# Attention with a sliding window and two MLPs on one core: the second set of weight combinations moves from POOL to VectorE and ACT, four products move between the last pairs' work, and VectorE takes sums first at changes of super-block

## The reference, cut to what matters

```python
# attention: 4 batches, 8 heads, 576 positions, head size 64
scores = scale * np.matmul(q, k.transpose(0, 1, 3, 2))
mask = (rel >= 0) & (rel < 128)
scores = np.where(mask, scores + bias[None], -1000000000.0)
attn = np.exp(scores - max); attn = attn / (sum + 1e-09)
x = np.matmul(attn, v)               # as 2304 tokens x 512
# first MLP: w_in 512 x 2048, w_out 2048 x 512
h = np.maximum(x @ w_in, 0.0); x = h * h @ w_out
# second MLP
h = x @ w_in; out = (h * np.cos(h)) @ w_out
```

## Time and profile before

| | before |
|---|---|
| median of 3 runs | 881.16 us (880.2 to 881.41) |
| the profiled execution's own time | 880.24 us |
| its span | 878.4 us |
| PE busy | 850.0 us (97%) |
| DVE busy | 645.3 us (73%) |
| ACT busy | 522.7 us (60%) |
| POOL busy | 96.1 us (11%) |
| granted clock of PE | 1.0 throughout |

### The profile page before, as it was taken

How to read it: one execution, slowest core, us unless ns; L and a number is a source line. 1 busy time by engine, 2 the same in 40 slices (tenths; PEclk the granted TensorE clock), 3 DMA queues, 4 the chain that set the end, 5 groups by cost and what they waited for, 6 DMA issues and landing times.

```text
span 878.4 us, 16151 instructions
## 1 busy us (share of the span) xinstructions
PE 850.0 (97%) x5840; PEld 766.0 (87%) x5840; DVE 645.3 (73%) x1437; ACT 522.7 (60%) x1141; POOL 96.1 (11%) x193
## 2 busy tenths in 40 slices
PE   6998789999999999999999999999999999999997
PEld 4887688999989999989999988898889889898986
DVE  6899577876767857777676687776777777767664
ACT  7888533433343433243342687887787877877774
POOL 7799900000000000000000000000000000000000
PEclk9999999999999999999999999999999999999999
DMA  6877506456588777777877556555575555565522
GB/s 211 254 236 264 184 12 229 155 209 239 181 293 297 235 283 287 276 243 284 297 265 256 190 194 202 183 163 187 187 264 181 168 190 192 204 224 183 192 72 72
DMA packets 72047, 185.34 MB, mean 211 GB/s; under 512 B 7200, under 2 KB 19488, under 8 KB 69920
## 3 DMA queue, kind: packets, MB, share of 16 engines
q1 hardware_dynamic: 71104, 183.23, 60.8%
q10 hardware_dynamic: 864, 1.08, 0.3%
HBM read 141.82 MB, written 42.47 MB: 210 GB/s over the span
## 4 chain that ended last, share of the span: by engine, by line
PE 87%; DVE 7%; issue 2%; POOL 2%; ACT 1%; DMA 0%; ACTq 0%; DVEq 0%; POOLq 0%
PE psum L699 38%; PE psum L733 22%; PE psum L738 14%; PE psum L740 7%; PE psum L642 2%; PE psum L554 2%; POOL probs L492 1%; PE psum L600 1%; DVE probs L1057 1%; DVE guarded L1066 1%; DVE g_lo L1231 1%; DVE hidden_sum L1177 1%; DVE pt L1077 1%; ACT probs L805 0%; DVE x L1101 0%
## 5 line engine op out<-in xcount | busy, mean ns | idle before, releaser
L699 PE MATMUL psum<-xt_hi,comb 128*128 128x384 f32 x1344 | 396.3, 337 | 6.2 <-DVE hidden_sum L1177 6.1
L699 PEld LDWEIGHTS psum<-xt_hi,comb 128*128 128x128 f32 x1344 | 247.4, 188 | 22.9 <-issue 8.2
L733 PE MATMUL psum<-wout,g_hi 128*128 128x512 f32 x576 | 180.5, 394 | 1.6 <-issue 1.3
L902 ACT ACTIVATE g_hi<-work 128x384 fp32r<-128x384 f32 x192 | 97.2, 518 | 95.2 <-DVE work L1226 53.9
L738 PE MATMUL psum<-g_hi,wout 128*128 128x512 f32 x384 | 149.7, 393 | 0.0
L1231 DVE TENSOR_TENSOR g_lo<-work,g_hi 128x384 fp32r<-128x384 f32 x192 | 102.1, 552 | 45.5 <-ACT g_hi L902 44.4
L699 PE MATMUL psum<-x_lo,comb 128*128 128x384 f32 x384 | 129.0, 336 | 0.0
L733 PEld LDWEIGHTS psum<-wout,g_hi 128*128 128x128 f32 x576 | 105.8, 188 | 14.6 <-issue 2.9
L733 PE MATMUL psum<-wout,g_lo 128*128 128x512 f32 x288 | 113.9, 395 | 0.0
L740 PE MATMUL psum<-g_hi,wout 128*128 128x256 f32 x384 | 107.9, 281 | 0.0
L699 PE MATMUL psum<-xt_lo,comb 128*128 128x384 f32 x288 | 96.9, 336 | 0.0
(11 more groups left out here) (101 smaller groups left out, 1292.7 us busy)
## 6 DMA issues: line engine op xcount, KB each, us to landing
comb<-comb SPq DMA_DIRECT2D x80, 768.0 KB, 4.9
wout<-wout SPq DMA_DIRECT2D x48, 512.0 KB, 4.9
comb<-comb SPq DMA_DIRECT2D x8, 1792.0 KB, 6.7
comb<-kept SPq DMA_DIRECT2D x8, 1792.0 KB, 7.4
wout_raw<-w_out SPq DMA_DIRECT2D x48, 256.0 KB, 4.4
comb<-comb SPq DMA_DIRECT2D x40, 256.0 KB, 3.1
v_raw<-v SPq DMA_DIRECT2D x16, 512.0 KB, 3.5
raw<-w_in SPq DMA_DIRECT2D x32, 256.0 KB, 6.9
```

The lines of the kernel that those rows point to most:

```text
L699: last = pe.matmul(psum[:, H_BANK + i % 2, 0:NH], wi, mi[:, k, :], start=first, stop=True, skip_group_check=True)
L733: last = pe.matmul(psum[:, Y_BANK + c, :], g[:, r, tok], w, start=start and m == 0, stop=True, skip_group_check=True)
L902: act.activation(g_hi[:, r, cols], work[i][:], ACT.Copy).then_inc(g_hi_ready, 1)
```

## The change

POOL makes only the first set of weight combinations, and spreads it over s = 6 to 12 with at most one part in each, the low part of the sums in two halves; its first token low part comes in s = 13 instead of 14. The second set is made by DVE (`weight_sums(1)`, `weights_lo(1)`, `sums_lo(1)` in s = 16, 17, 18) and ACT (`weights_hi(1)`, `sums_hi(1)` in s = 16, 17). ACT rounds T4 and B22 one step earlier. PE has products 0 to 3 of step 0 between the transposes of pairs 14 and 15. Step 0 on DVE has its own order (`very_first_step`). In steps 1, 9 and 17 DVE makes the sums first and `weights_lo`, `sums_lo`, `kept_wout_lo` and `moving_sum` later, and in steps 2 to 6 `split_at` comes last but one. In the second MLP `lo_g(n - 1, 2)` comes ahead of the copies of a finished block when n % 8 = 1.

```diff
+FIRST_HI = {12: ["B11"], 13: ["T3"], 14: ["T2"], 15: ["T1"], 16: ["B21", "T4"], 17: ["B22"]}
 FIRST_PAIRS = [8, 12, 16]
...
-            def first_sums_lo(n):
-                pool.wait_ge(comb_hi_ready, 2 * n + 2)
-                pool.tensor_tensor(comb[:, n, 1, 3:7, :], sums[:], comb[:, n, 0, 3:7, :].bitcast(F32),
-                                   ALU.subtract).then_inc(comb_ready, 1)
+            def first_sums_lo(a):
+                pool.wait_ge(comb_hi_ready, 2)
+                last = pool.tensor_tensor(comb[:, 0, 1, a + 3:a + 5, :], sums[:, a:a + 2, :],
+                                          comb[:, 0, 0, a + 3:a + 5, :].bitcast(F32), ALU.subtract)
+                if a == 2:
+                    last.then_inc(comb_ready, 1)
...
                 normalise(s - 1)
-                n, part = divmod(s - LATE_LOADS - 2, 4)
-                if 0 <= n < 2:
-                    (first_weight_sums, first_weights_hi, first_weights_lo, first_sums_lo)[part](n)
-                if s >= FIRST_T + 3 and s - FIRST_T - 3 < len(MOVING):
-                    first_moving_lo(s - FIRST_T - 3)
-            for i in range(PAIRS - FIRST_T - 2, len(MOVING)):
+                if s == POOL_WEIGHTS:
+                    first_sums(False)
+                elif s == POOL_WEIGHTS + 1:
+                    first_sums(True)
+                elif s == POOL_WEIGHTS + 2:
+                    first_weights_hi()
+                elif s == POOL_WEIGHTS + 3:
+                    first_sums_hi()
+                elif s == POOL_WEIGHTS + 4:
+                    first_weights_lo()
+                elif s == POOL_WEIGHTS + 5:
+                    first_sums_lo(0)
+                elif s == POOL_WEIGHTS + 6:
+                    first_sums_lo(2)
+                elif s > POOL_WEIGHTS + 6:
+                    first_moving_lo(s - POOL_WEIGHTS - 7)
+            for i in range(PAIRS - POOL_WEIGHTS - 6, len(MOVING)):
                 first_moving_lo(i)
 
...
-                if s < PAIRS:
-                    all_scores(s)
-                else:
-                    values(s - 3)
-                    if s == PAIRS:
-                        pe.wait_ge(biased, UNITS * PAIRS)
-                    if s < PAIRS + 2:
-                        hidden_product(0, s - PAIRS)
+            for s in range(PAIRS):
+                all_scores(s)
                 if s == 2:
                     pe.wait_ge(pool_consts, 2)
-                if 2 <= s < PAIRS + 2:
+                if s >= 2:
                     transposes(s - 2, 0)
                     transposes(s - 2, 1)
-                if 3 <= s < PAIRS:
+                if s >= 3:
                     values(s - 3)
-                if 2 <= s < PAIRS + 2:
+                if s >= 2:
                     transposes(s - 2, 2)
                     transposes(s - 2, 3)
-            for i in range(2, len(PRODUCTS)):
+            values(PAIRS - 3)
+            transposes(PAIRS - 2, 0)
+            transposes(PAIRS - 2, 1)
+            pe.wait_ge(biased, UNITS * PAIRS)
+            hidden_product(0, 0)
+            transposes(PAIRS - 2, 2)
+            transposes(PAIRS - 2, 3)
+            hidden_product(0, 1)
+            values(PAIRS - 2)
+            transposes(PAIRS - 1, 0)
+            transposes(PAIRS - 1, 1)
+            hidden_product(0, 2)
+            transposes(PAIRS - 1, 2)
+            transposes(PAIRS - 1, 3)
+            hidden_product(0, 3)
+            values(PAIRS - 1)
+            for i in range(4, len(PRODUCTS)):
                 hidden_product(0, i)
             pe.wait_ge(x_ready, PAIRS)
...
-                copy_first_sum(n)
+                    copy_first_sum(n)
                 if n > 0:
                     round_g(n - 1, 3)
...
-                if FIRST_T + 1 <= s < FIRST_T + 1 + len(MOVING):
-                    round_moving(0, SPLIT_ORDER[s - FIRST_T - 1])
+                for name in FIRST_HI.get(s, ()):
+                    round_moving(0, name)
                 if s == PAIRS:
                     copy_part(0)
+                    weights_hi(1)
+                elif s == PAIRS + 1:
+                    copy_first_sum(0)
+                    sums_hi(1)
             for n in range(FRESH):
                 first_step(n)
             for n in range(FRESH, ALL + 1):
...
+                make_g(0, 0)
+                c22_sum(0)
+                make_g(0, 1)
+                c21_sum(0)
+                make_g(0, 2)
+                lo_g(0, 0)
+                c12_sum(0)
+                make_g(0, 3)
+                lo_g(0, 1)
+                moving_sum(1, "T3")
+                split_wout(1)
...
             def first_step(n):
                 t, j = divmod(n, STEPS)
-                job = job_of(n)
+                job, turn = job_of(n), j == 1
                 if job is not None and n % 2 == 0:
                     kept_weight_sums(job)
-                if n > 0:
-                    part_b_sum(n)
-                    lo_g(n - 1, 2)
-                if j == 1 and t > 0:
+                part_b_sum(n)
+                lo_g(n - 1, 2)
+                if turn and t > 0:
                     put_y(t - 1)
                 if makes_weights(n):
                     weight_sums(n + 1)
                 if job is not None and n % 2 == 0:
                     kept_weights_lo(job)
-                if n > 0:
-                    lo_g(n - 1, 3)
-                    split_wout(2 * n - 2)
-                split_at(n)
+                lo_g(n - 1, 3)
+                split_wout(2 * n - 2)
+                if not makes_weights(n):
+                    split_at(n)
                 part_c_sum(n)
-                if makes_weights(n):
+                if makes_weights(n) and not turn:
                     weights_lo(n + 1)
                 make_g(n, 0)
-                if T_AT[j]:
+                if T_AT[j] and not turn:
                     moving_sum(t + 1, T_AT[j])
                 c22_sum(n)
                 make_g(n, 1)
                 if makes_weights(n):
-                    sums_lo(n + 1)
+                    (weights_lo if turn else sums_lo)(n + 1)
                 if job is not None and n % 2 == 0:
                     kept_sums_lo(job)
-                elif job is not None:
+                elif job is not None and not turn:
                     kept_wout_lo(job)
                 c21_sum(n)
                 make_g(n, 2)
...
                 lo_g(n, 1)
                 c12_sum(n)
                 make_g(n, 3)
+                if turn:
+                    if makes_weights(n):
+                        sums_lo(n + 1)
+                    else:
+                        kept_wout_lo(job)
+                    moving_sum(t + 1, T_AT[j])
+                if makes_weights(n):
+                    split_at(n)
                 split_wout(2 * n + 1)
 
             def second_step(n):
...
                     turn_low(n - 1, 3)
+                    if j == 1:
+                        lo_g(n - 1, 2)
                     if n < ALL:
                         if j == 1:
                             (put_out(t - 1, False) if t > SUPERS else put_y(t - 1))
                         split_at(n)
-                    lo_g(n - 1, 2)
+                    if j != 1:
+                        lo_g(n - 1, 2)
                 if n < ALL:
                     part_c_sum(n)
...
                     copy_pt(s - 3, 3)
+                if s == PAIRS + 1:
+                    part_b_sum(0)
+                elif s == PAIRS + 2:
+                    part_c_sum(0)
                 if s < PAIRS:
                     for n, u in enumerate(ORDER[0:5]):
                         bias_scores(s, n, u)
@@ -1352,9 +1411,14 @@
                     copy_x(s - 3)
                 if FIRST_T <= s < FIRST_T + 4:
                     moving_sum(0, ["T3", "T1", "T2", "T4"][s - FIRST_T])
-                if s == PAIRS + 1:
-                    part_b_sum(0)
-            for n in range(FRESH):
+                if s == PAIRS:
+                    weight_sums(1)
+                elif s == PAIRS + 1:
+                    weights_lo(1)
+                elif s == PAIRS + 2:
+                    sums_lo(1)
+            very_first_step()
+            for n in range(1, FRESH):
                 first_step(n)
             for n in range(FRESH, ALL + 1):
                 second_step(n)
```

48 lines of the change are left out of this document (26 added, 22 removed).

## The result

| | before | changed |
|---|---|---|
| median | 880.75 us (879.93 to 881.41, 6 runs) | 885.08 us (883.86 to 887.10, 6 runs) |
| the profiled execution's own time, its span | 880.24, 878.4 us | 886.29, 884.5 us |
| PE busy, matmuls | 850.0 us, 5840 | 856.3 us, 5840 |
| DVE, ACT, POOL busy | 645.3, 522.7, 96.1 us | 647.9, 523.7, 88.1 us |
| granted clock, mean | 1.0 | 0.992 |

The ratio is 1.0053, with a 95% interval of 1.0039 to 1.0066: the change makes the kernel 4.3 us slower. A second measurement of the same kernel, in ten executions, gave 1.0024 (experiment 8), so the size of the loss varies. The prediction was 877.4, within 871.5 to 882.0, with a chance of 0.08 for slower. It was wrong.

What follows compares the result with a forecast made beforehand. PE, busy 97% of the span, was taken to bound the kernel. Seven terms sum to -3.25 us from the profiled 880.24, giving 877.0, or 877.9 by the median; forecast 877.4, range 871.5 to 882.0.

Steps and rivals of the forecast that it cites:

- term 1: POOL's ten slots from s = 6 to the start of s = 16: 57.8 us instead of 61.5, 3.7 less.
- term 2: SP's queue: pair 15's k load lands 2.8 late for its scores, PE regains part: 1.1 us more.
- Term 3: Pair 13's values to step 1, with products between the last pairs: 21.3 us instead of 23.25, 1.95 less.
- Term 4: Last pairs, DVE's second-set sums beside POOL: one wait for a low part of 1.84, and 0.3: 2.1 us more.
- Rival 3: End of attention: pair 14's copy waits for two POOL low parts, pair 15's for a third; 883.9 us, chance 0.07.
- The prediction's own sign for a time above 880: End of the attention: a PE wait over 2 us at pair 14's or 15's values.
- term 6: Steps 9 and 17: reordering wins 3.0, but a later store landing delays steps 10 and 18: net 2.6 us lost.
- term 5: Step 1: the waits of 0.89 and 0.30 for DVE's sums go, with the slower restart: 1.6 us less.
- Term 7: Second MLP: the three waits of "issue" at the changes of block go: 1.8 us less.

Runs made afterwards that it cites:

- experiment 8: Changed kernel measured again: 883.57 us, ratio 1.0024; then changed kernel with the second MLP's `lo_g(n - 1, 2)` back behind the output copies: 888.16 us, one execution.
- experiment 6's first run: The three edits, kept weights' sums later in all even steps, second set's sums behind pair 14's last copy, POOL waiting for them: 881.92 us, ratio 1.0015.
- experiment 3: Changed kernel with the first weight set's store and the load behind it on SP's queue after pair 15's q and k: 885.92 us, ratio 1.0057.
- experiment 4, second run: The three edits with steps 9 and 17 also put back in the order of the kernel before: 874.14 us, ratio 0.9916.
- Experiment 6: Second run: the best version with the second set's sums behind pair 14's last copy and the first partial sum, no POOL wait: 875.07 us, ratio 0.9928.
- experiment 7: Kernel before with useless DVE writes, growing in number, ahead of one sum in steps 11, 13, 15, 19 and 21: 901.97 us, one execution.
- the three edits: Changed kernel with POOL waiting for the second set's sums, kept sums behind the first partial sum (steps 10, 18), store after pair 15's loads: 875.88 us, ratio 0.9943.
- the best version: The three edits with the expert weights', tokens' and left-over low parts ahead of the kept weights' sums in steps 10 and 18 alone: 871.79 us, ratio 0.9892.

## Why the prediction was wrong

By its own terms, against the profiled executions' spans (+6.1):

| term | forecast | measured |
|---|---|---|
| start, clock at the lower level for longer | 0 | +0.93 |
| 1 and 2, POOL's slots, k's load | -2.6 | -2.22 |
| 3 and 4, last pairs, DVE beside POOL | +0.15 | +3.66 |
| 5, step 1 | -1.6 | -0.72 |
| 6, steps 9 and 17 | -3.0 | -3.14 |
| 6, steps 10 and 18 | +5.6 | +8.00 |
| 7, second MLP | -1.8 | -0.46 |
| sum | -3.25 | +6.05 |

- **The start** is no part of the change, whose first edit stands in s = 6; the clock rose at 16.41 instead of 8.39. In the other profiled executions pair 0's values stand 0.2 to 1.6 behind before's, the most in the seven that have a fall at 17, behind a wait of 2.1 to 2.2 for the first probabilities. Before and experiment 6's first run have that wait (2.11, 2.10) and no fall.
- **Terms 1 and 2** are right. POOL's ten slots take 58.85 us (37.81 to 96.66) against 57.8 forecast and 61.5 before. Between pair 0's and pair 13's values the seven executions with the edit of experiment 3 gain 3.3 to 3.4 on before (term 1: 3.7), and the changed kernel 2.2; so the late k costs 1.1, as term 2 says, though PE waits 1.43 for it where 2.8 was forecast. With a fall behind that wait it costs 2.1 and 2.5 (experiment 8).
- **Term 3** is right by itself: where POOL is out of the way (experiment 4, second run) the stretch takes 1.66 less than before; forecast 1.95.
- **Term 4 is the first of two steps that failed.** It took "one wait for a low part of 1.84, and 0.3", 2.1. In the profile it is 1.61 + 1.49 for the third and fourth sum and 1.40 for the weights' low part, 4.5; its upper end was 4. The reason given for one wait, that the fourth sum waits for the third and so lets POOL in, holds for both, since POOL had a queue of ready low parts. The rule of the Trainium skill that the prediction quoted (SBUF — State Buffer, section "SBUF: two separate sides": whoever starts first holds the ports for its whole instruction) says a whole low part at each place, and the trace agrees with it and not with the 0.1 per instruction read off the token sum. Experiment 6 goes beyond it: 4.56 for one instruction, over three of POOL's. Rival 3 had this mechanism, with its two low parts ahead of pair 14's copy and one ahead of pair 15's, and 883.9; it had 0.07. The prediction's own sign for a time above 880, a PE wait over 2 us at pair 14's values, came.
- **The second step that failed is the clock: it was no term and no rival.** Before shows 1.77 as its longest wait behind the start of step 0 and no fall, and I took the cost of a wait to be its length and 0.17. Without a fall steps 10 and 18 cost 2.67, 2.82 and 2.95 over before in three executions, the 2.8 of **term 6**; with one they cost 4.00 in the mean of seven, so a fall costs 1.2 there. In step 1 it is 1.5: from its first product to step 4 the time is 2.26 less than before without a fall (the run with the odd order back) and 0.72 less with one; forecast 1.6 less, **term 5**, which by itself was 0.7 too small.
- **Term 6** was right in its mechanism and its size up to the clock: DVE's sums start at 266.97 once the store has landed; forecast 265.3 on a scale where step 9 stands 1.65 earlier. That its first half is borrowed was said; that DVE has other work ready for the gap, worth 3.7 us a place with the fall, was not seen.
- **Term 7** took the next wait to be nothing, or the bank's copy. It is neither: ahead of steps 26 and 34 PE now waits 0.44 and 0.49 for a sum of DVE, which it does not do with the old order (experiment 8), these steps take what they took, and one place of three gains.

So of the 9.3 us between forecast and profile, 3.5 are at the last pairs, with one fall in them, 2.4 are two falls at steps 10 and 18, 0.9 are step 1 (a fall of 1.5, which hides a gain of 0.7 over term 5), 1.3 term 7, 0.9 the start, and 0.3 the rest. Counted by cause, two falls at steps 10 and 18 (2.4), one in step 1 (1.5), one behind pair 14's wait (some 1.2, as at steps 10 and 18) and the late start (0.9) make 6.0 us of clock. That is more than term 4, which without its fall is some 2.3 above the forecast, but it is term 4 and the store of term 6 that made three of the waits. Without the 6.0 the profiled execution would have come to some 880.3, inside the range; both are estimates from the figures above. The medians differ by less, 4.3, since the profiled execution of after is 1.2 above its median and that of before 0.5 below its own.

What stays open: why a wait of 2.1 to 2.4 is followed by a fall in one execution and not in another, and why a fall came behind the two waits of 0.8 and 1.3 at the end of step 0 in five profiled executions (the changed kernel's, the three edits', the best version's among them) and not in seven others with the same two waits. Not tried: the best version with the odd steps put back.

## What to carry to other kernels

When two-input work moves to DVE beside a POOL with a queue of SBUF work, count a whole POOL instruction for each place where POOL can start first, and put a POOL wait there if DVE's result is the urgent one: here a wait on the less urgent engine was worth 4 to 7 us. Look at what lies behind a reordered store before counting the gain, and fill the engine's gap until it lands with what is ready. Price a wait of TensorE that is longer than any in the profile before with the matmuls behind it at half clock; here a fall behind a wait cost between 1 and 2 us more than the wait. Compare two profiles from the same point behind the start, since the start varied by 1.6 us with no edit to it.

## What the hardware showed that I had not expected

A DVE sum of two SBUF inputs, 0.42 alone, lasted 2.03 and 1.91 beside single POOL instructions, and 4.56 beside three in a row (5.4 us of POOL's work); the other way round, a POOL low part of 1.84 beside a DVE one that had begun 0.3 earlier lasted 2.56. Copies from PSUM (0.41) and sums with a PSUM input (0.54) that started beside POOL's low parts kept their length.

The granted clock fell to its lower level behind 7 of the 10 waits for `part_b` of 2.08 to 2.36 in five profiled executions, behind neither of 2.14 and 3.12 in experiment 7, behind one of 2.65, and behind or in all seven waits from 3.39 to 6.52 later than the start; two of five waits of 1.43 to 1.85 for k were followed by one as well, and seven of nine from 2.10 to 2.22 for the first probabilities. The length of a wait alone does not decide. The Trainium skill, TensorE: Matmul & The Clock Gate, Part 1, says that a TensorE at rest goes back to the lower clock and that the hardware's observation runs free of the kernel's own start, so that the point of the change varies. The spread between executions agrees, and so does the clock's first rise, which the records place between 6.8 and 16.5 us; no run here could move that phase on purpose.
